# A reordered attention head with filler products, and the first batch's v summed on chip

## What is computed

```
q_d, k_d, v_d = mean over groups of 4 tokens          # 144 pooled tokens
out_d     = softmax(q_d k_d^T / 8) v_d ;  out_up = repeat(out_d, 4)
out_local = softmax(q k^T / 8 where |i-j| < 4) v
x = (out_up + out_local) as 2304 tokens x 512
y = ((x w_a) * (x w_b)) w_out                         # 512 -> 1536 -> 512
h = y w_in ; s = h*softmax(h) ; out = (layernorm(s)*g_ln) w_out2
```

## Time and profile before

| | |
|---|---|
| time, median of 3 | 786.36 us (786.12 to 787.45) |
| the profiled execution: time, span | 787.3 us, 785.5 us |
| first dense product starts | 47.26 us |
| TensorE busy: whole span, from 100 us on | 760.1 us (97%), 673.9 of 685.5 us |
| VectorE, ScalarE, GpSimd busy | 71%, 38%, 27% |
| DMA moved | 109.41 MB |

### The profile page before, as it was taken

How to read it: one execution, slowest core, us unless ns; L and a number is a source line. 1 busy time by engine, 2 the same in 40 slices (tenths; PEclk the granted TensorE clock), 3 DMA queues, 4 the chain that set the end, 5 groups by cost and what they waited for, 6 DMA issues and landing times.

```text
span 785.5 us, 12293 instructions
## 1 busy us (share of the span) xinstructions
PE 760.1 (97%) x4440; PEld 699.4 (89%) x4440; DVE 559.7 (71%) x977; ACT 298.4 (38%) x819; POOL 211.2 (27%) x264
## 2 busy tenths in 40 slices
PE   6999999898999999999999999999999999999998
PEld 5778899798999999998999999999988888888886
DVE  4589999979868987778777876122467767666663
ACT  3544747263353535353424424234322212222222
POOL 3468898355423330051001111122100000000000
PEclk9999999999999999999999999999999999999999
DMA  9999846586788575582755433536121011011011
GB/s 185 216 226 229 199 119 198 153 260 186 228 206 228 145 206 172 161 221 70 215 146 169 135 106 111 194 115 215 54 67 51 30 55 52 29 55 51 30 41 41
DMA packets 86573, 109.41 MB, mean 139 GB/s; under 512 B 20081, under 2 KB 53361, under 8 KB 86513
## 3 DMA queue, kind: packets, MB, share of 16 engines
q1 hardware_dynamic: 71792, 99.12, 46.9%
q10 hardware_dynamic: 14721, 9.51, 4.3%
HBM read 87.76 MB, written 20.84 MB: 138 GB/s over the span
## 4 chain that ended last, share of the span: by engine, by line
PE 77%; POOL 2%; DMA 1%; issue 0%; ACT 0%; SPq 0%
PE psum L872 24%; PE psum L874 24%; PE psum L873 24%; PE psum L985 2%; PE psum L829 1%; POOL raw L1723 1%; DMA raw<-in_q 1%; PE psum L809 1%; PE psum L840 1%; PE psum L819 1%; POOL raw L1727 1%; PE psum L791 0%; ACT out_sb L1283 0%; ACT out_d L1099 0%; SPq L510 0%
## 5 line engine op out<-in xcount | busy, mean ns | idle before, releaser
L872 PE MATMUL psum<-x_hi,w_hi 128*128 128x384 f32 x576 | 199.3, 346 | 2.6 <-POOL w_lo L1735 1.6
L874 PE MATMUL psum<-x_hi,w_lo 128*128 128x384 f32 x576 | 194.2, 337 | 0.0
L873 PE MATMUL psum<-x_lo,w_hi 128*128 128x384 f32 x576 | 194.1, 337 | 0.0
L872 PEld LDWEIGHTS psum<-x_hi,w_hi 128*128 128x128 f32 x576 | 109.3, 190 | 6.9 <-issue 3.7
L873 PEld LDWEIGHTS psum<-x_lo,w_hi 128*128 128x128 f32 x576 | 109.3, 190 | 0.0
L874 PEld LDWEIGHTS psum<-x_hi,w_lo 128*128 128x128 f32 x576 | 109.1, 189 | 0.0
L1411 DVE TENSOR_TENSOR ab_f<-psum,a_sb 128x384 f32<-128x384 f32 x72 | 39.9, 554 | 93.5 <-PE psum L874 63.2
L872 PE MATMUL psum<-ab_hi,wo_hi 128*128 128x384 f32 x288 | 101.4, 352 | 3.4 <-issue 3.4
L874 PE MATMUL psum<-ab_hi,wo_lo 128*128 128x384 f32 x288 | 98.2, 341 | 0.0
L873 PE MATMUL psum<-ab_lo,wo_hi 128*128 128x384 f32 x288 | 98.1, 341 | 0.0
L1723 POOL TENSOR_TENSOR raw<-raw 96x256 f32<-96x256 f32 x60 | 56.2, 962 | 120.1 <-DMA raw<-in_q 54.6
(11 more groups left out here) (148 smaller groups left out, 1422.9 us busy)
## 6 DMA issues: line engine op xcount, KB each, us to landing
wo_hi<-wo_hi_scratch SPq DMA_DIRECT2D x53, 256.0 KB, 2.7
wo_lo<-wo_lo_scratch SPq DMA_DIRECT2D x53, 256.0 KB, 3.2
wo_raw<-in_moe_w_out SPq DMA_DIRECT2D x19, 256.0 KB, 4.3
raw<-in_v SPq DMA_DIRECT2D x8, 576.0 KB, 7.7
yT_scratch<-y_sb ACTq DMA_DIRECT2D x6, 768.0 KB, 6.5
y_raw<-yT_scratch SPq DMA_DIRECT2D x18, 256.0 KB, 3.0
out<-out_sb SPq DMA_DIRECT2D x18, 256.0 KB, 2.1
k_u<-in_k SPq DMA_DIRECT2D x11, 384.0 KB
```

Of the source, the lines that this page charges most:

```text
L872: mm(dst, wh, xh, start=first, stop=False, skip_group_check=not check)
L873: mm(dst, wh, xl, start=False, stop=False, skip_group_check=not check)
L874: last = mm(dst, wl, xh, start=False, stop=end, skip_group_check=not check)
```

## The change

The head's order is rewritten on all engines. TensorE gets `keep_busy(n, count)`: `count` products of 128x128 by 128 columns, in float32, whose result nobody reads, in a bank that is free at that point. They are 39 in all, 26 of them from the one ahead of `head_turn_p(0)` on. VectorE fills their operand first (`ones_ready`).

The v of batch 0 is no longer summed by rows and sent through DRAM: `load_raw_v` loads it with a pooled key on each of 72 partitions, `pool_v(c)` sums it on GpSimd straight into `v_d`, with one signal per pair. `head_up(c)` waits for its own pair. SyncE loses two stores and one load, and its order changes: w_out block 0 and batch 1's v rows go ahead of `q_u` and `k_u`; `v_u` of unit (1, 0) is loaded before tile 0; in tile 0, weights 3 go behind k's rows and w_out block 3.

Two jobs of tile 0 move from slots 12 and 17 to 15 and 20, the transposes of k's and q's sums from 10 and 11 to 12 and 14, the first turns of x from 22 to 25, `load_xup` from 18 to 20. The local steps get a buffer of their own, `part`, in place of `accT`; the wait for `x_turned` goes to the last step.

```diff
-JOBS = [(0, 0, "R", 0, 0), (0, 5, "R", 0, 2), (0, 12, "R", 1, 0), (0, 17, "R", 1, 2),
+JOBS = [(0, 0, "R", 0, 0), (0, 5, "R", 0, 2), (0, 15, "R", 1, 0), (0, 20, "R", 1, 2),
-QK_AT = {0: {10: (4, 5), 11: (6, 7)}, ...
+QK_AT = {0: {12: (4, 5), 14: (6, 7)}, ...
-    first, second = 22 if m in (0, 3) else 17, 32 if m == 0 else 31
+    first, second = (25, 17, 17, 22, 17)[m], 32 if m == 0 else 31
 SyncE
+            def load_raw_v():
+                for x in range(2):
+                    sp.dma_start(raw_v[:, x].rearrange("p y c e -> p (y c) e"),
+                                 bass.AP(v.tensor, x * SH * R4 * D, [[R4 * D, SH], [S * D, H], [1, R4 * D]])
+                                 ).then_inc(s.raw_v_loaded, 16)
-            load_raw(0, 2, 0)
-            load_raw(0, 2, 1)
+            load_raw_v()
             load_weights(0)
+            load_wo(0)
+            load_raw(1, 2, 0)
+            load_raw(1, 2, 1)
             load_unit_q(1, 0)
             load_unit_k(1, 0)
-            store_vd(0, 0)
-            store_vd(0, 1)
-            load_vd(0)
-            load_raw(1, 2, 0)
-            load_raw(1, 2, 1)
-            load_wo(0)
             load_wo(1)
...
+            sp.wait_ge(s.v_summed, PPB)
+            load_unit_v(1, 0)
...
-                    if m == 0 and j in (1, 3, 5):
-                        load_weights((j + 5) // 2)
                     if m == 0 and j == 1:
                         load_raw(1, 1, 0)
                         load_raw(1, 1, 1)
+                    if m == 0 and j in (2, 3, 5):
+                        load_weights((j + 5) // 2 if j > 2 else 3)
 TensorE
+            def keep_busy(n, count):
+                for _ in range(count):
+                    mm(bank(n, 128), xup[:, 0, :], xup[:, 1, :], start=True, stop=True)
...
-                if c == 0:
-                    pe.wait_ge(s.vd_loaded, 16)
+                pe.wait_ge(s.v_summed, c + 1)
...
+            pe.wait_ge(s.ones_ready, 1)
+            keep_busy(5, 6)
             head_turn(0)
+            keep_busy(5, 2)
...
             head_turn(2)
+            keep_busy(5, 3)
             head_turn_p(0)
             head_scores(2)
-            head_values(0)
             head_turn(3)
             head_turn_p(1)
+            keep_busy(5, 2)
+            head_values(0)
...
+            pe.wait_ge(s.x_local, 2)
+            keep_busy(5, 6)
             head_values(2)
+            keep_busy(3, 2)
+            head_turn_p(3)
...
+            pe.wait_ge(s.x_local, 3)
+            keep_busy(5, 2)
             head_values(3)
             head_up(0)
             head_up(1)
+            pe.wait_ge(s.hp_pT_ready, 1)
+            keep_busy(7, 8)
...
+            keep_busy(GA, 3)
             up_product(0, 0, WA)
 VectorE
-                slots = [acc[:, :, :], tmp[:, 1], tmp[:, 0], tmp[:, 2], turned_slot, tmp[:, 2], turned_slot]
+                slots = [acc[:, :, :], tmp[:, 1], tmp[:, 0], tmp[:, 2], part[:, :, :], tmp[:, 2], part[:, :, :]]
...
-                    if e == 4:
-                        at_least(dve, s.x_turned, 2 * (u - 2))
...
                     dve.wait_ge(s.xup_loaded, 32 * (u - 1))
+                    at_least(dve, s.x_turned, 2 * (u - 2))
 GpSimd
+            def pool_v(c):
+                if c == 0:
+                    pool.wait_ge(s.raw_v_loaded, 32)
+                for x in range(2):
+                    t = raw_v[:, x, :, c, :]
+                    last = G.tensor_tensor(t[:, :, 0:128], t[:, :, 0:128], t[:, :, 128:256], ALU.add)
+                last.then_inc(s.v_step, 1)
+                pool.wait_ge(s.v_step, c + 1)
+                for x in range(2):
+                    t = raw_v[:, x, :, c, :]
+                    last = G.tensor_tensor(v_d[:, c, x, :].rearrange("p (y d) -> p y d", y=2),
+                                           t[:, :, 0:D], t[:, :, D:2 * D], ALU.add)
+                last.then_inc(s.v_summed, 1)
             normalise(0)
             normalise(1)
-            pool_rows(0, 2, 0)
-            pool_rows(0, 2, 1)
             normalise(2)
+            pool_v(0)
             normalise(3)
+            pool_v(1)
+            pool_v(2)
+            pool_v(3)
...
-                    if m == 0 and j in (1, 2):
-                        pool_rows(1, 1, j - 1)
+                    if m == 0 and j in (2, 3):
+                        pool_rows(1, 1, j - 2)
```

More of the change, by code:

```diff
@@ L222, in build_program @@
     accT = place("accT", [128, TPP, HPP * D], FP32)
+    part = place("part", [128, HPP, TPP * D], FP32)
     xup = place("xup", [128, TPP, HPP * D], FP32)
     raw = [place(f"raw{i}", [PPB * BLK, 2, 3, R4 * D], FP32) for i in range(2)]
-    raw_head = [place(f"raw{2 + i}", [PPB * BLK, 2, 3, R4 * D], FP32, o) for i, o in enumerate((v_at, acc_at))]
+    raw_v = place("raw_v", [SH, 2, 2, PPB, R4 * D], FP32, v_at)
     raw_x = {1: [place(f"raw{6 + i}", [PPB * BLK, 2, 3, R4 * D], FP32, o + 4 * DC * NT)
@@ L335, in loads_to @@
         return sum(unit_loads(w // 2, w % 2, before, count) for w in range(2, u + 1))
-    POOL_SUMS = [(b, tau, half) for b, taus in ((0, (2,)), (1, (2, 0, 1)), (2, (2, 0, 1)), (3, (2, 1, 0)))
+    POOL_SUMS = [(b, tau, half) for b, taus in ((1, (2, 0, 1)), (2, (2, 0, 1)), (3, (2, 1, 0)))
                  for tau in taus for half in range(2)]
@@ L376, in build_program @@
         wos_names = [f"wo_stored{i}" for i in range(SLOTS)]
-        raw_names = [f"raw_loaded{i}" for i in range(10)]
+        raw_names = [f"raw_loaded{i}" for i in range(6)]
         qh_names = [f"q_h_loaded{c}" for c in range(PPB)]
@@ L411, in raw_buffer @@
                 return raw[half], raw_loaded[half], 16 * (RAW_PASS.index((b, tau)) + 1)
[L412 to L414 removed]
+            return raw_x[b][half], raw_loaded[1 + b + half], 16
         def pooled_rows(t, i):
@@ L465, in load_raw @@
                     if tau2 == 2:
-                        sp.wait_ge(vd_stored[half], 16 * (b2 + 1))
+                        sp.wait_ge(vd_stored[half], 16 * b2)
                     else:
@@ L586, in tile @@
                             rest = m in (0, 3)
-                            if m == 0 and n == 3:
-                                load_unit_v(1, 0)
                             if n == (11 if m == 0 else 4):
@@ L824, in pooled_values @@
                 pe.wait_ge(s.pT_out, i + 1)
-                pe.wait_ge(s.vd_loaded, 16 * (JOBS[i][3] + 1))
+                if JOBS[i][3] == 0:
+                    pe.wait_ge(s.v_summed, PPB)
+                else:
+                    pe.wait_ge(s.vd_loaded, 16 * JOBS[i][3])
                 for h in range(2):
@@ L1231, in _ @@
             head_pooled_pT(1)
+            head_pooled_exp(2)
+            head_pooled_exp(3)
+            weight_high(0)
             head_pooled_pT(2)
@@ L1429, in _ @@
             heads3 = [128, HPP, TPP, D]
-            turned_slot = accT[:, :, :].rearrange("p t n -> p (t n)").rearrange("p (h x) -> p h x", h=HPP)
             def local_step(m, g, step, marks, used):
```

51 lines of the change are left out of this document (25 added, 26 removed).

## The result

The changed kernel takes **792.22 us** (median of 4 runs, 792.0 to 792.83) against 786.24 us (4 runs, 785.58 to 787.45) in the same session: a ratio of 1.0073, 95% interval 1.0057 to 1.0089. It is slower; the forecast was 780.8 us and the range ended at 787.0. The profiled execution took 792.39 us, its span is 790.8.

What follows compares the result with a forecast made beforehand. VectorE was taken to set tile 0's end, with TensorE nearly full afterwards, so gate 2's time counts. Gate 2 5.6 us earlier: 787.3 - 5.6 = 781.7 profiled, median 0.9 lower, 780.8 us; range 775.0 to 787.0.

Steps and rivals of the forecast that it cites:

- The DMA sum: Head: 576 KB less (2.4 us) and no pause (1.8 us) bring batch 1's q rows from 53.27 to 49.1 us.
- the bad bound: Head: if v's shorter pieces eat 2.4 us of DMA, q's first half lands at 51.5 us.
- Rival C: Head: DMA not relieved, q's rows still at 53, gate 2 about 72, time 785 to 787; chance 0.13.
- The v sums: GpSimd in the head: four pairs take 9.6 us instead of about 7, ending near 36, ahead of q's rows.
- From q's sums to block 2: Tile 0: q's sums run 49.1 to 58.6 us, nearly contended; TensorE starts block 2 1.45 us later, at 60.0.
- The clock: Block 2: after the longer wait TensorE's dense products run slow, costing 2.5 us, at most 3.6.
- Gate 2: VectorE's gate after block 2's up products: at 67.7 us against 73.31, 5.6 earlier; bounds 8.7 and 0.8 us earlier.
- VectorE's 70.89 us left as they are: Gate 2 to half 1's `accT`: same steps, same GpSimd work beside them, so the stretch stays 70.89 us.
- nothing of its own: Tile 0: moved jobs, turns and QK transposes cost nothing, inside VectorE's 70.24 busy us, unless TensorE became the bound.
- A gain at gate 2 taken whole to the end: Tile 0 onward: the 5.6 us won at gate 2 come off the total time in full.
- A: Tile 0: VectorE stalls less, TensorE bounds without a wait at the end, gain 10.2 us, time 776.2; chance 0.20.
- B: Head: array stays at 1.2 GHz, fillers stand in the path, first dense product past 51.6, time 790.9; chance 0.15.

Runs made afterwards that it cites:

- novd: Kernel before, without the two stores and the load of batch 0's pooled v (`v_d` holds zeros for it): ratio 0.9994, 784.39 us.
- split_slots: Changed kernel with v loads cut at 64 and 8 partitions, k's sums back in blocks 1 and 2, and tile 0's old slots: 0.9989, 784.55 us.
- split_rows: Changed kernel with v loads cut at 64 and 8 partitions and k's sums back in blocks 1 and 2, slots still moved: 1.0003, 785.88 us.
- after_split: Changed kernel with each of the two v loads cut at 64 and 8 partitions, nothing else: 1.0033, 788.25 us.
- rowsback: Changed kernel with only GpSimd's sums of batch 1's k moved back to blocks 1 and 2: ratio 1.0063.
- nofill: Changed kernel with all 39 filler products left out and every wait kept: 1.0092, 792.15 us.
- after_lowfirst: Changed kernel with GpSimd making block 2's low part ahead of batch 1's q sums and block 3's between their halves: 1.0042, 788.31 us.
- oldrows: Changed kernel with batch 0's v rows loaded in the old form, 96 partitions and 3 KB pieces: 1.0026, 787.25 us.
- slotsback: Changed kernel with k's sums back in blocks 1 and 2 and tile 0's jobs, transposes, turns and `load_xup` in old slots: 1.0072.

## Why the prediction was wrong, by its steps

**The DMA sum: the step that failed.** The 4.2 us for 576 KB and the pause were nearly right (3.43 by themselves in novd). The term beside it, the new form of the v load, was bounded by nothing and 2.4 us from the one aspect looked at, the length of the pieces; in the same place as the old form it costs 56.17 - 48.91 = 7.3 us. q's rows landed at 56.17, past the bad bound of 51.5. Of the 7.3 us, 4.2 go with the number of partitions, 72 carried by twelve engines as inferred above: with 64 + 8 q's sums start at 51.96, near that bound. The other 3 are open. Rival C had this side of it right, that the DMA would not be relieved, but put q's rows at 53 and was too cheap.

**The v sums.** 9.6 us forecast, 9.6 measured (the eight groups of `pool_v`). v landed at 27.94 instead of 25, and the first dense product was at 41.37, in the forecast 37 to 42.

**From q's sums to block 2.** 9.5 us taken (49.1 to 58.6; 10.7 was the contended bound), 65.43 - 56.17 = 9.3 measured; then 1.45 us as forecast. The wait of 9.12 us lies in the forecast 6 to 12 by luck: the first product came some 4 us later than thought and the rows 7 us later.

**The clock.** 2.5 us forecast; block 2's products took 74.79 - 66.88 = 7.91 us against 5.19, 2.7 more.

**Gate 2**, 67.7 forecast, was at 74.95: 7.2 us of the 10.7 by which the profiled time missed 781.7.

**VectorE's 70.89 us left as they are.** Failed, by 3.6 us. The prediction gave "nothing of its own" to the moved jobs and QK transposes, and in time that holds (split_slots against split_rows: 0.9989 and 1.0003, intervals overlapping), but not for its reason: the work is not "all inside VectorE's 70.24 busy us", since TensorE became the bound. And it passed over the last hunk of the diff, k's sums one block later on GpSimd, behind weights of a block that was itself late: 4.74 us at slot 14, with half speed behind it (the dense products from 102.32 on are 0.32 us apart). Moved back on time, they shorten the stretch by 3.0 us (split_rows against after_split). The stall of 5.48 us at 99.98 lies in this stretch too; what it costs by itself no run tells. That mending this wait pays showed only once q's rows were in time; rowsback alone gained nothing clear.

**A gain at gate 2 taken whole to the end.** No run bears it out. In novd gate 2 is 2.6 us earlier and the time is the same within 1.6 us; in split_rows it is 2.0 us earlier and the ratio is 1.0003. So even with q's rows in time the 5.6 us are not shown to be there to win.

**The rivals.** A came in its first half: VectorE was busy 65.12 us in place of 70.24 and had 8.5 to spare, and TensorE bounded tile 0. But no gain followed, since TensorE was busy longer (67.85 us against 65.24) and waited for k's sums, and its sign, no wait at the end of the tile, did not show (2.45 us). B's time, 790.9, is near the measured one, but its mechanism is not: the first dense product was not past 51.6 us but at 41.37, and nofill is no faster. Judged by the time alone, B would have been right by luck.

## What to carry to other kernels

When a load changes its form, look at its partitions first and its pieces second: here, as inferred, 72 partitions left four of sixteen DMA engines ahead, and what came late was not that load but one issued 24 us later. A part that "only moves" on a busy engine must be followed to the one that waits for it, every hunk of it. An engine that was full before a change need not be full after it: look at its share of the stretch again, before a gain is carried through it. And time won by putting GpSimd's work in another order can go again in stalls of VectorE beside it and in waits for what now comes later: in after_lowfirst 3.3 of 7.6 us did not reach the end of the tile.

## What the runs showed of the hardware

- Behind transfers over 72 or 36 partitions the packets came out of step (32 of 128 packets ahead, the first of them 4.3 and 5.2 us before the first of the rest). At a DMA share over 1.0 the rate was 183 to 189 KB/us there and 223 to 245 in the kernel before and oldrows: here a full share did not tell the rate.
- VectorE instructions that take 0.95 to 1.5 us elsewhere took 5.5 and 8.23 us beside GpSimd work without a gap. The Trainium skill, page SBUF — State Buffer, section "SBUF: two separate sides", describes a lock that is held for one instruction of the other engine, which blocks meanwhile; the trace agrees that VectorE is held up, but over some thirteen GpSimd instructions on end (87.78 to 96.0).
- Fillers of full size raised the clock within the head, in most runs: the dense products at 41.62 and 41.79 stand 0.17 us apart, 2.4 GHz, and the first took 0.41 us. It took that in eight of the fourteen profiles with fillers and 0.66 in all six without. After waits of 0.78, 0.83 and 0.24 us for `x_lo` they were 0.32 apart again from 45.77 on. In five more heads with fillers, after_split and oldrows among them, the first dense product took 0.67 us, in slotsback 0.54.
